# Building the decay mask from the powers' rows in SBUF instead of through DRAM

## The reference

```
rel    = pos[:, None] - pos[None, :]                   # inside a block
Dmask  = where(rel >= 0, lam ** rel, 0)                # per head
intra  = (q_b @ k_b^T * Dmask) @ v_b
inter  = (q_b * lam ** (pos + 1)) @ state
out_b  = intra + inter
state  = lam ** block * state + (k_b * lam ** (block - 1 - pos))^T @ v_b
```

## Time and profile before

| | us |
|---|---|
| median of 3 runs | 540.8 |
| lowest, highest | 538.77, 544.58 |
| the profiled execution | 541.94 |
| its span (first to last instruction) | 540.2 |
| TensorE busy | 521.1 (96%) |
| GpSimd, VectorE, ScalarE busy | 222.6, 215.6, 204.9 |
| TensorE's mean granted clock | 0.988 of full |

### The profile page before, as it was taken

The page is one execution under the profiler, slowest core; times in us unless marked ns, Lnnn a source line. Parts: engine busy times, 40 slices in busy tenths (PEclk is TensorE's granted clock), DMA queues, the critical chain, the costliest instruction groups (busy, mean ns, idle before and its releaser), DMA issues. The chain is left out here.

```text
span 540.2 us, 9225 instructions
## 1 busy us (share of the span) xinstructions
PE 521.1 (96%) x3000; PEld 430.0 (80%) x3001; DVE 215.6 (40%) x417; ACT 204.9 (38%) x352; POOL 222.6 (41%) x236
## 2 busy tenths in 40 slices
PE   7899999999999999999999999999989999999994
PEld 6778888888778888878888888878878888888873
DVE  3443332333335422223533566462222472222892
ACT  0143343333343344444334556222222552222880
POOL 2675554554322556444245735041121161112461
PEclk8899999999999999999999999999999999999997
DMA  5954434430020530006400000205873101111110
GB/s 175 400 225 157 147 128 156 152 83 9 0 79 2 184 127 0 0 0 224 165 0 1 0 1 27 91 23 167 261 254 136 39 21 39 39 39 39 39 36 2
DMA packets 23161, 49.54 MB, mean 92 GB/s; under 512 B 8919, under 2 KB 10591, under 8 KB 23136
## 3 DMA queue, kind: packets, MB, share of 16 engines
q1 hardware_dynamic: 16496, 41.83, 21.9%
q0 software_dynamic: 2896, 7.36, 4.4%
q10 hardware_dynamic: 3744, 0.03, 0.4%
HBM read 42.80 MB, written 7.20 MB: 93 GB/s over the span
## 5 line engine op out<-in xcount | busy, mean ns | idle before, releaser
L523 POOL TENSOR_TENSOR wi_lo<-wd_raw,wi_hi 128x512 fp32r<-128x512 f32 x48 | 62.2, 1296 | 145.1 <-ACT wi_hi L670 145.0
L1264 PE MATMUL psum<-xT,wi_lo 128*128 128x512 f32 x192 | 77.3, 402 | 0.0
L1272 PE MATMUL psum<-wo_hi,act_lo 128*128 128x512 f32 x192 | 75.7, 394 | 1.3 <-DVE act_lo L922 1.3
L1266 PE MATMUL psum<-xT,wi_hi 128*128 128x512 f32 x192 | 75.0, 391 | 0.0
L1265 PE MATMUL psum<-xT,wi_hi 128*128 128x512 f32 x192 | 74.9, 390 | 0.0
L1274 PE MATMUL psum<-wo_hi,act_hi 128*128 128x512 f32 x192 | 74.8, 390 | 0.0
L1273 PE MATMUL psum<-wo_lo,act_hi 128*128 128x512 f32 x192 | 74.7, 389 | 0.0
L919 DVE SCALAR_TENSOR_TENSOR act_f<-psum,act_f 128x512 f32<-128x512 f32 x48 | 33.1, 690 | 97.2 <-ACT act_f L688 96.7
L688 ACT ACTIVATE act_f<-psum 128x512 f32<-128x512 f32 x48 | 28.6, 597 | 97.3 <-PE psum L1266 94.1
L528 POOL TENSOR_TENSOR wo_lo<-wd_raw,wo_hi 128x512 fp32r<-128x512 f32 x48 | 61.9, 1289 | 2.7 <-ACT wo_hi L675 2.7
L1353 PE MATMUL psum<-we_hi,he_lo 128*128 128x512 f32 x120 | 48.4, 403 | 2.4 <-DVE he_lo L1013 2.0
(11 more groups left out here) (170 smaller groups left out, 832.3 us busy)
## 6 DMA issues: line engine op xcount, KB each, us to landing
we_raw<-w_exp SPq DMA_DIRECT2D x32, 512.0 KB, 4.9
wd_raw<-w_dense SPq DMA_DIRECT2D x16, 512.0 KB, 5.8
qk_in<-attn_qk SPq DMA_DIRECT2D x10, 512.0 KB, 3.4
kv_in<-attn_kv SPq DMA_DIRECT2D x10, 512.0 KB, 3.4
x_d<-x_sb SPq DMA_DIRECT2D x12, 256.0 KB, 2.3
qk_more<-attn_qk SPq DMA_DIRECT2D x2, 512.0 KB, 7.1
kv_more<-attn_kv SPq DMA_DIRECT2D x2, 512.0 KB, 7.8
decay_mask<-pow_d SPq DMA_DIRECT2D x2, 256.0 KB, 3.6
```

The costliest lines, as they stand in the source:

```text
L523: nc.gpsimd.tensor_tensor(wi_lo[:, r, :], dense_raw(f, 0), wi_hi[:, r, :].bitcast(F32), ALU.subtract).then_inc(s_wil, 1)
L1264: nc.tensor.matmul(h, w_lo, hi, start=(c == 0), stop=False)
L1266: mm = nc.tensor.matmul(h, w_hi, hi, start=False, stop=(c == DC - 1))
L1272: nc.tensor.matmul(bank(ACC + i), lo, wo_hi[:, r, :], start=first, stop=False)
```

## The change

The tensor in DRAM and the write to it are gone. Eight transfers, one per head, copy the windows of one row of `pw` in SBUF to the 128 partitions of the mask: SP issues heads 0, 1, 4 and 5, ACT heads 2, 3, 6 and 7. The queries and keys of chunk 1 are issued after SP's four, not before. The mask's two semaphores now count four transfers each. The query decay comes from TensorE: a small tile `of_head` (8 rows x 4 pairs x 128), made by GpSimd, has a one where the row is the head of that output partition; four matmuls with it, placed behind the scores of chunk 0, spread the rows of `pw` to 128 partitions in PSUM bank 7, and ACT copies the bank to `q_decay`. TensorE waits for that copy ahead of the second warm-up, which has 11 matmuls instead of 13.

```diff
-WARM = (6, 13)
+WARM = (6, 11)
...
-        pow_d = nc.dram_tensor("pow_d", [H, PWW], F32).ap()
...
+        of_head = place("of_head", [H, PAIRS, P], F32)
...
+        def spread_mask(eng, h):
+
+            row = pw[h:h + 1, 1:2]
+            eng.dma_start(decay_mask[:, h, :], bass.AP(tensor=row.tensor, offset=row.offset, ap=[list(row.ap[0]), [1, P], [1, P]])
+                          ).then_inc(s_mask[h % 2], 16)
...
             load_qk(0, 0)
             load_kv(0, 0)
+
+            sp.wait_ge(s_pow, 1)
+            for h in (0, 1, 4, 5):
+                spread_mask(sp, h)
             load_qk(1, 1)
-
-            sp.wait_ge(s_pow, 1)
-            sp.dma_start(pow_d, pw[:]).then_inc(s_pow_d, 16)
-            sp.wait_ge(s_pow_d, 16)
-            for half in range(2):
-                sp.dma_start(decay_mask[:, half::2, :], bass.AP(tensor=pow_d.tensor, offset=half * PWW + 1,
-                                                                ap=[[1, P], [2 * PWW, PAIRS], [1, P]])).then_inc(s_mask[half], 16)
-            for hp in range(2):
-                sp.dma_start(q_decay[hp * D:(hp + 1) * D],
-                             bass.AP(tensor=pow_d.tensor, offset=hp * PWW + P + 1,
-                                     ap=[[0, D], [2 * PWW, PAIRS], [1, P]])).then_inc(s_tables, 16)
             load_kv(1, 1)
...
             nc.gpsimd.memset(ident[:], 0.0).then_inc(s_chain, 1)
+            nc.gpsimd.memset(of_head[:], 0.0).then_inc(s_head, 1)
...
+            pool.wait_ge(s_head, 1)
+            for hp in range(2):
+                nc.gpsimd.affine_select(out=of_head[:, :, hp * D:(hp + 1) * D], in_=of_head[:, :, hp * D:(hp + 1) * D],
+                                        compare_op=ALU.not_equal, fill=1.0, base=-hp,
+                                        pattern=[[-2, PAIRS], [0, D]], channel_multiplier=1).then_inc(s_head, 1)
...
-                pool.wait_ge(s_mask[half], 16)
+                pool.wait_ge(s_mask[half], 16 * PAIRS)
...
-            pool.wait_ge(s_tables, 32)
+            pool.wait_ge(s_tables, 1)
...
         def _(act):
+            act.wait_ge(s_pow, 1)
+            for h in (2, 3, 6, 7):
+                spread_mask(act, h)
+            act.wait_ge(s_qp, 1)
+            nc.scalar.activation(q_decay[:].rearrange("p a n -> p (a n)"), bank(7), ACT.Copy).then_inc(s_tables, 1)
...
-                        dve.wait_ge(s_mask[half], 16)
+                        dve.wait_ge(s_mask[half], 16 * PAIRS)
...
             scores(0, 0, 16, score_bank(0))
+            pe.wait_ge(s_head, 3)
+            pe.wait_ge(s_pow, 1)
+            for hp in range(PAIRS):
+                mm = nc.tensor.matmul(bank(7)[:, hp * P:(hp + 1) * P], of_head[:, hp, :], pw[:, P + 1:2 * P + 1], start=True, stop=True)
+            mm.then_inc(s_qp, 1)
...
                 if n == 0:
+                    pe.wait_ge(s_tables, 1)
                     warm(WARM[1])
```

More of the change, by code:

```diff
@@ L248, in fused_program @@
         s_pow = sem("powers_made")
-        s_pow_d = sem("powers_in_dram")
         s_mask = [sem(f"decay_mask_loaded{i}") for i in range(2)]
-        s_tables = sem("query_decay_loaded")
+        s_qp = sem("query_decay_spread")
+        s_tables = sem("query_decay_ready")
+        s_head = sem("head_select_made")
         s_fill = sem("scratch_filled")
```

## The result

The changed kernel takes 557.66 us (median of 4 runs, 556.1 to 560.1) against 540.9 before (4 runs, 538.77 to 544.58). The ratio is 1.031, with a 95% interval of 1.024 to 1.038. The profiled execution took 556.1 us, with a span of 554.4 against 540.2. Further down, two executions at a mean granted clock of about 0.75 (655.11 us of the kernel before, 650.19 us of the version without transfers) are left out of the medians and the ratios.

The account below looks back on a forecast made before the run. TensorE was taken as the bound from the first dense matmul on. Chunk 2's scores 0.1 us earlier and no low spell (-1.5) made it start 1.6 us earlier: 540.0 us; own case 537 to 543, full range to 559.

Parts of the forecast that it names:

- the slow port: Mask reads from SBUF: neighbouring partitions share one port at 27.1 GB/s, two groups in turn; about 556 us, chance 0.27.
- The masks in by 10.0: Eight mask transfers: SBUF rows read as fast as DRAM rows, all landed at 10.0, 3.2 us earlier than 13.22.
- both ends: Mask reads: 3.2 us earlier at the DRAM row's pace, or 19.3 us of reading at one DMA engine's 27.1 GB/s.
- The first rival: Mask reads through one port after another: landing near 26.2, queries at 27.5, chunk 0's end 34.2, +15 us; chance 0.27.
- Its milder form: Both row groups read side by side: masks landed at 16.6, queries at 17.9, +5.4 us, 547; chance 0.08.
- Chunk 1's queries at 10.9: SP's load moved behind the masks: issued at 7.07, landing at 10.9 against 8.34 before.
- Query decays: Four TensorE matmuls in the first hole, 0.73 us, then ACT's copy of 0.60, ending before 8.0.
- GpSimd: Head-select rows: 0.7 us in all, at most 0.2 ahead of the identity, nothing on the path.
- The filler: Warm-up matmuls before chunk 0's attention, cut from 13 to 11: 3.55 us, between 2.0 and 3.7.
- The second hole: TensorE's idle time from chunk 0's end at 15.69 to chunk 2's data at 17.72, expected to go.
- chunk 1's slow spell: Low clock after the second hole, costing chunk 1 about 1.5 us, expected to go: -1.5.
- What bounds the kernel: TensorE sets the time from the first dense matmul at 31.58; changes to its start carry to the end one for one.

Follow-up runs that it names:

- the version without transfers: Kernel before, with mask and query decays made by exp on ACT, loads issued without waits, second warm-up of 4 matmuls: 535.4 us against 540.4, ratio 0.992.
- the moving starts: Changed kernel with all windows of a head starting at the row's first number, not moving on by 4 bytes each: 529.49 us, not comparable (mask all zeros).
- both groups: Changed kernel with SP issuing heads 0 to 3 and ACT heads 4 to 7, so both groups of four partitions are read at once: 550.06 us.
- the same queues on one group: Changed kernel with SP on heads 0 to 3, ACT on 4 to 7, but all masks read from rows on partitions 0 to 3: 558.59 us.
- eight spread rows: Changed kernel with powers made on 128 partitions, 16 per head; SP reads partitions 0, 16, 36, 52, ACT 64, 80, 100, 116: 549.98 us.
- the run with the queries first: Changed kernel with chunk 1's queries and keys issued before SP waits for the powers, as in the kernel before: 551.98 us.
- The part alone: Kernel before with only the query decays spread by TensorE and copied by ACT, 13 warm-up matmuls kept: 538.71 us against 540.4, ratio 0.999.
- the last run: Mask and query decays by exp on ACT, second warm-up cut from 4 matmuls to 1: 535.38 us against 541.52 for the kernel before, ratio 0.990.

## Why the prediction was wrong

It said 540.0, no change, at 0.62, and gave the slow port 0.27. The measured 557.66 lies inside the range, which reached to 559 for that rival's sake, but on the side that I held for less likely.

**The masks in by 10.0: the step that failed.** I had both ends, the DRAM row's pace and one engine's pace, and took the first "since it is the same packets into the same tile". The packets are the same at the receiving end only. The second half was used at 26.46, and the rate of 24 to 25 GB/s is the other end of my bound, 27.1, less what the moving starts cost (27 without them). Two runs show it as a property of the source: 57 GB/s with both groups, 25 with the same queues on one group; and the DRAM source alone restores 13.2 of 15.65 us. The Trainium skill's rule that I had set beside the sum ("SBUF — State Buffer", "Door 1: The DMA port swizzle") gave the right sum; the trace of the changed kernel agrees with it for reads too, and so do the 57 GB/s of two groups. More outlets than two are not borne out that well: eight spread rows gave a mean of 63. The nearest row was near in packet size and far in what mattered, where the bytes leave from.

**The first rival, as it was worked out:** landing near 26.2 (26.46), chunk 1's queries at 27.5 (27.61), chunk 0's end at 34.2 (35.06), +15 (15.65). Its mechanism and its size were right; the chance was mis-set. That the landing fits to 0.3 us is luck: the transfers were issued at 4.55 and not 5.19, the rate was 24 to 25 GB/s up to 14 and not 27.1, and from 16 to 18 it was 47: three misses that nearly cancel. Its milder form, both groups side by side, was given 17.9 for the queries; the run that does it shows 19.18.

**Chunk 1's queries at 10.9.** Wrong with the masks, and for a reason that no rival named: the issues themselves block. SP's four masks took 9.68 us and not 1.9, so the load was not queued at 7.07 behind the masks but issued at 14.28. For this load it made little difference, since its data had to wait for the masks either way: the rival, without blocking, had it at 27.5. What is left with the masks' source put back is 2.4 us; undoing the order of loads in the changed kernel gave back 4.9.

**Query decays.** The four matmuls took 2.07 us, not 0.73, within the hole. The copy on ACT, priced as over before 8.0, ended at 17.8, behind ACT's 11.32 us of issues and a table load of 1.28 that the sum had left out (it now stands between the issues and the copy); the late queries hid it, and the run with the queries first lays it bare as a wait of 8.34 us. The part alone costs nothing (0.999).

**GpSimd.** At most 0.2 us was allowed ahead of the identity; its select started at 2.03 instead of 1.58. It stayed hidden, as argued.

**The filler** took 3.94 us for 22 records, above my 3.7: TensorE's matmuls were slow after the long hole (11 records in the 2 us from 30 to 32, shown at the end). **The second hole and chunk 1's slow spell** went, as said: -1.61 against -1.5.

**What bounds the kernel** was right: what the head lost or won came out at the end, 15.65 against 14.2 in the span, and 8.6 us won in the head of the last run against 8.9 in its span (531.3). One for one holds for these single profiles; between medians the last run won 6.1 us, and the changed kernel lost 16.8.

## What to carry to other kernels

A transfer has two ends: before a bounce through DRAM is removed, ask through how many partitions the bytes leave SBUF, for rows of four neighbouring partitions gave out 25 GB/s together, a tenth of the rate at which the same packets, beside those of the query decays, ran from DRAM. A slow transfer also blocks the queue that issues it and what else that engine does, so don't put bulk issues ahead of compute on ACT. Where a table is a function of position, an engine that idles in the head can make it (2.44 us of ACT here for 524 KB), and the loads that follow no longer wait.

## What the runs showed that I had not expected

- An issue can take long: 4.90 and 5.45 us for one load on SP while slow transfers of the same queue were outstanding, 0.43 from 24.71 on.
- The time until a small write is seen grows with the loads ahead of it on the shared engines: 1.5, 3.5, 4.25 and 6.1 us for the same 8 KB.
- The granted clock does not always tell TensorE's pace. In the changed kernel it reads 1.00 from 30 to 32 us, yet only 11 records were done in those 2 us, as few as at 0.50 before (6 in 1 us); the scores behind the long hole took 2.08 us both there and in the run with both groups, where the clock reads 0.50. The matmuls that spread the query decays took 2.07 us in the changed kernel and 1.15 in the run with both groups, with the clock at 1.00 in both.

```profile
30.00:32.00 2.00, 2.00 (x11) 2.00 (x11) 1.05 (x2) 0.00 (x0) 1.06 (x1) 1.00 0.95 371
```
